# A fused attention and feed-forward kernel: own product copied ahead of the casts, weight casts moved from GpSimd to ScalarE, the product by value from VectorE to GpSimd

## The reference

```python
def reference(q, k, v, tau, moe, moe2):
    qn = q / (norm(q, axis=tokens) + 1e-6); kn = k / (norm(k, axis=tokens) + 1e-6)
    a = softmax(kn.T @ qn / tau)            # 256 x 256
    x = v @ a                               # 6016 x 256
    xn = x / rms(x) * rms_g
    g, val = xn @ w_gate, xn @ w_val        # 256 -> 1536
    y = (g * sigmoid(g) * val) @ w_out      # 1536 -> 256
    h = y @ w_in                            # 256 -> 2048
    return (h - tanh(h)) @ w_out2           # 2048 -> 256
```

## Time and profile before

| | us |
|---|---|
| median of 3 runs (lowest, highest) | 1223.22 (1222.99, 1223.24) |
| profiled execution | 1223.24, its span 1221.4 |
| PE busy | 1179.6 (97%), weight loads 989.7 (81%) |
| VectorE busy | 963.3 (79%) |
| ScalarE busy | 455.1 (37%) |
| GpSimd busy | 262.1 (21%) |
| ScalarE: cast of 512 columns, mean (L861); of 1024 (L743) | 0.611; 1.050 |
| VectorE: low part of 512 columns, mean (L1258) | 0.712 |
| VectorE: seven unit's product by value, mean (L1214); shortest and longest | 1.000; 0.548 and 1.494 |
| GpSimd: gate product (L721), shortest and longest | 1.009 and 1.795 |
| GpSimd: cast of 1024 columns, mean (L714) | 1.225 |
| load of combined weights, 1 MB, from issue to landing, median | 5.3 |

### The profile page before, as it was taken

The page is one execution under the profiler, slowest core; times in us unless marked ns, Lnnn a source line. Parts: engine busy times, 40 slices in busy tenths (PEclk is TensorE's granted clock), DMA queues, the critical chain, the costliest instruction groups (busy, mean ns, idle before and its releaser), DMA issues.

```text
span 1221.4 us, 18368 instructions
## 1 busy us (share of the span) xinstructions
PE 1179.6 (97%) x5858; PEld 989.7 (81%) x5858; DVE 963.3 (79%) x1760; ACT 455.1 (37%) x775; POOL 262.1 (21%) x208
## 2 busy tenths in 40 slices
PE   9999999999999999998999999999999899999999
PEld 8888887877877887887887787788788778888898
DVE  6888797886977877788697697778878869778776
ACT  7866424233322423423332332342342333234232
POOL 4610002042033014113203302401410430330220
PEclk9999999999999999999999999999999999999999
DMA  9524544061043024005104202501510520320300
GB/s 371 188 74 117 146 109 142 1 173 69 1 129 111 0 74 133 33 8 164 69 0 137 103 0 86 155 0 17 187 36 0 163 74 0 121 104 1 91 31 14
DMA packets 132790, 104.83 MB, mean 86 GB/s; under 512 B 90640, under 2 KB 112784, under 8 KB 132752
## 3 DMA queue, kind: packets, MB, share of 16 engines
q1 hardware_dynamic: 132320, 103.83, 27.2%
q10 hardware_dynamic: 432, 0.52, 0.1%
HBM read 91.88 MB, written 12.45 MB: 85 GB/s over the span
## 4 chain that ended last, share of the span: by engine, by line
PE 69%; DVE 15%; issue 7%; ACT 4%; POOL 1%; DMA 1%; DVEq 1%; ACTq 1%; SPq 0%
PE ring L1505 29%; PE out_acc L1563 20%; PE y_acc L1563 6%; PE ring L1556 5%; DVE act L1214 4%; DVE h_lo L1258 2%; PE out_acc L1489 2%; DVE act L1163 2%; PE ring L1521 2%; DVE w_in L1190 2%; PE y_acc L1424 2%; DVE gate_pair L1195 2%; ACT gate_pair L868 1%; PE y_acc L1434 1%; POOL act L721 1%
## 5 line engine op out<-in xcount | busy, mean ns | idle before, releaser
L836 ACT ACTIVATE act<-ring 128x512 f32<-128x512 f32 (+1 forms) x273 | 159.9, 587 | 296.9 <-PE ring L1505 269.3
L1258 DVE TENSOR_TENSOR h_lo<-act,h_hi 128x512 fp32r<-128x512 f32 (+1 forms) x336 | 235.0, 712 | 8.0
L1505 PE MATMUL ring<-y_hi,wl 128*128 128x512 f32 (+1 forms) x712 | 241.2, 385 | 0.0
L1563 PE MATMUL out_acc<-h_hi,wl 128*128 128x512 f32 x704 | 240.0, 389 | 0.3 <-DVE h_lo L1258 0.3
L721 POOL TENSOR_TENSOR act<-gate_pair,act 128x512 f32<-128x512 f32 (+1 forms) x60 | 80.6, 1344 | 732.6 <-ACT act L873 732.6
L714 POOL CAST wl<-landing 128x1024 fp32r<-128x1024 f32 x120 | 143.5, 1225 | 155.6 <-DMA landing<-combined 155.6
L1173 DVE TENSOR_TENSOR act<-ring,act 128x512 f32<-128x512 f32 (+1 forms) x192 | 128.8, 671 | 55.8 <-ACT act L836 54.9
L1563 PEld LDWEIGHTS out_acc<-h_hi,wl 128*128 128x128 f32 x704 | 132.1, 188 | 28.5 <-DVE h_lo L1258 0.7
L1505 PEld LDWEIGHTS ring<-y_hi,wl 128*128 128x128 f32 x712 | 133.4, 188 | 25.6
L1505 PE MATMUL ring<-y_lo,wl 128*128 128x512 f32 (+1 forms) x356 | 137.0, 385 | 0.0
L1563 PE MATMUL out_acc<-h_lo,wl 128*128 128x512 f32 x352 | 136.9, 389 | 0.0
(11 more groups left out here) (230 smaller groups left out, 2014.4 us busy)
## 6 DMA issues: line engine op xcount, KB each, us to landing
landing<-combined SPq DMA_DIRECT2D x60, 1024.0 KB, 5.3
out_dram<-out_rows SPq DMA_DIRECT2D x88, 64.0 KB, 1.8
qk_in<-in_k_dram SPq DMA_DIRECT2D x9, 512.0 KB, 8.8
qk_in<-in_q_dram SPq DMA_DIRECT2D x9, 512.0 KB, 9.8
v_in<-in_v_dram SPq DMA_DIRECT2D x72, 64.0 KB, 2.3
w_in<-in_moe_w_out_dram SPq DMA_DIRECT2D x12, 256.0 KB, 3.0
combined<-wl SPq DMA_DIRECT2D x12, 256.0 KB, 4.2
combined<-w_in SPq DMA_DIRECT2D x12, 256.0 KB, 3.2
```

The lines of the kernel that those rows point to most:

```text
L836: nc.scalar.activation(act[:, u % RING, 0:width], bank(t, name)[:, 0:width], func).then_inc(act_ready, 1)
L1258: nc.vector.tensor_tensor(h_lo[:, u % RING, 0:width], act[:, u % RING, 0:width], f32(h_hi[:, u % RING, 0:width]), ALU.subtract).then_inc(h ...
L1505: ins = nc.tensor.matmul(bank(t, name)[:, 0:width], weights(c, w_part), (hi if part else lo)[:, c, 0:width], start=c == 0 and w_part and part,
L1563: ins = nc.tensor.matmul(acc[:, d, 0:width], weights, (h_hi if part else h_lo)[:, u % RING, 0:width], start=f == 0 and w_part and part, st ...
```

## The change

Three things move.

1. In `seven_unit` ScalarE copies the own product first and casts units p-2 and p-1 after it; until now the cast of the seven unit stood ahead of the next pair's copy. Only in the last pair is the seven unit's cast still behind the sigmoid of the plain unit.
2. `mark_seven` goes from GpSimd to ScalarE, as one instruction over both planes, one seven unit ahead instead of two, between the casts and the sigmoid of `gate_pair`. The first block is cast after tile 1. TensorE waits for one increment instead of two.
3. GpSimd multiplies by gate and then by value (`finish_seven`), and signals `seven_made`. VectorE's second sum (value0) waits for `seven_made` of the pair before, as it overwrites `value_pair`. In the last pair VectorE makes both products itself, ahead of the plain unit's.

```diff
-        PRODUCTS, STEPS, T_STEPS = 7, 8, 4
+        PRODUCTS, STEPS, T_STEPS = 7, 7, 4
+
+        LAST_SEVEN = 2 * SEVENS - 2
...
-            def mark_seven(t, j):
-
-                n = j % len(SEVEN_BLOCKS)
-                pool.wait_ge(seven_loaded[n], t * 32 + (16 * (j // len(SEVEN_BLOCKS) + 1) - 32 * SEVEN_FROM))
-                for low in range(2):
-                    nc.gpsimd.tensor_copy(wl[:, low, SEVEN_BLOCKS[n], :],
-                                          landing[:, low, SEVEN_BLOCKS[n], :]).then_inc(seven_ready, 1)
-
-            def gate_seven(t, p):
+            def finish_seven(t, p):
                 width = width_of(t)
                 buf = act[:, p % RING, 0:width]
                 pool.wait_ge(act_ready, t * U + p + 1)
                 nc.gpsimd.tensor_tensor(buf, gate_pair[:, 0:width], buf, ALU.mult).then_inc(seven_gated, 1)
...
+                pool.wait_ge(seven_gated, sevens(t, p, 1, 1))
+                pool.wait_ge(seven_step, sevens(t, p, STEPS, BY_VALUE0))
+                nc.gpsimd.tensor_tensor(buf, value_pair[:, 0:width], buf, ALU.mult).then_inc(seven_made, 1)
+
+            for t in range(SEVEN_FROM, TILES):
+                for p in range(0, LAST_SEVEN, 2):
+                    finish_seven(t, p)
...
             def cast_any(t, u, width):
 
-                act_e.wait_ge(seven_step, sevens(t, u, STEPS, STEPS)) if u % 2 == 0 else \
+                if u % 2 == 0:
+                    act_e.wait_ge(seven_made, sevens(t, u, 1, 1))
+                else:
                     act_e.wait_ge(bank_free, freed(t, ("value", u)))
...
-            def seven_unit(t, p, width):
+            def mark_seven(t, j):
+
+                n = j % len(SEVEN_BLOCKS)
+                act_e.wait_ge(seven_loaded[n], t * 32 + (16 * (j // len(SEVEN_BLOCKS) + 1) - 32 * SEVEN_FROM))
+                nc.scalar.copy(wl[:, :, SEVEN_BLOCKS[n], :], landing[:, :, SEVEN_BLOCKS[n], :]).then_inc(seven_ready, 1)
+
+            def seven_unit(t, p, width, last):
                 half = width // 2
                 act_e.wait_ge(seven_full, sevens(t, p, PRODUCTS, OWN))
                 if p > 0:
                     act_e.wait_ge(seven_gated, sevens(t, p))
                 nc.scalar.copy(gate_pair[:, 0:half], bank(t, ("own", p))[:, 0:half]).then_inc(own_copied, 1)
-                if p > 0:
-                    cast_any(t, p - 1, width)
+                for u in range(max(p - 2, 0), p):
+                    cast_any(t, u, width)
+                if p < LAST_SEVEN:
+                    mark_seven(t, p // 2 + 1)
+                elif not last:
+                    mark_seven(t + 1, 0)
                 act_e.wait_ge(seven_step, sevens(t, p, STEPS, BY_GATE1))
...
-                        if not is_plain(t):
+                        if not is_plain(t) and f == G - 1:
                             cast_any(t, f - 1, width)
...
             first_tile()
             tile(1, False)
+            mark_seven(SEVEN_FROM, 0)
...
                 dve.wait_ge(seven_full, sevens(t, p, PRODUCTS, SUM3))
+                if p > 0:
+
+                    dve.wait_ge(seven_made, sevens(t, p))
                 nc.vector.tensor_tensor(value0, of("sum3"), u2, ALU.add).then_inc(seven_step, 1)
...
-            def seven_value(t, p, width):
+            def finish_seven(t, p, width):
                 buf = act[:, p % RING, 0:width]
+                dve.wait_ge(act_ready, t * U + p + 1)
+                nc.vector.tensor_tensor(buf, gate_pair[:, 0:width], buf, ALU.mult).then_inc(seven_gated, 1)
                 dve.wait_ge(seven_gated, sevens(t, p, 1, 1))
                 dve.wait_ge(seven_step, sevens(t, p, STEPS, BY_VALUE0))
-                nc.vector.tensor_tensor(buf, value_pair[:, 0:width], buf, ALU.mult).then_inc(seven_step, 1)
+                nc.vector.tensor_tensor(buf, value_pair[:, 0:width], buf, ALU.mult).then_inc(seven_made, 1)
...
                         seven_sums(t, f, width, lambda: low_before(f))
                         beside(f)
+                        if f == LAST_SEVEN:
+                            finish_seven(t, f, width)
                         continue
                     buf = act[:, f % RING, 0:width]
-                    if is_plain(t):
-                        gate_times(t, f, buf, width)
-                    else:
-                        ending = f == G - 1
-                        if ending:
-                            gate_times(t, f, buf, width, lambda: seven_value(t, f - 1, width))
-                            low_unit(t, f - 1, width)
-                        else:
-                            gate_times(t, f, buf, width)
-                            seven_value(t, f - 1, width)
+                    gate_times(t, f, buf, width)
+                    if not is_plain(t) and f == G - 1:
+                        low_unit(t, f - 1, width)
...
-                        pe.wait_ge(seven_ready, sevens(t, f, 2, 2))
+                        pe.wait_ge(seven_ready, sevens(t, f, 1, 1))
```

More of the change, by code:

```diff
@@ L343, in build @@
         seven_gated = sem("seven_gated")
+        seven_made = sem("seven_made")
         seven_step = sem("seven_step")
@@ L721, in gate_seven @@
                 nc.gpsimd.tensor_tensor(buf, gate_pair[:, 0:width], buf, ALU.mult).then_inc(seven_gated, 1)
-            for j in range(len(SEVEN_BLOCKS)):
-                mark_seven(SEVEN_FROM, j)
-            MARKED = len(SEVEN_BLOCKS)
-            for n in range(SEVENS * (TILES - SEVEN_FROM)):
-                gate_seven(SEVEN_FROM + n // SEVENS, 2 * (n % SEVENS))
-                if n > 0:
-                    ahead = n - 1 + MARKED
-                    if ahead < SEVENS * (TILES - SEVEN_FROM):
-                        mark_seven(SEVEN_FROM + ahead // SEVENS, ahead % SEVENS)
+                pool.wait_ge(seven_gated, sevens(t, p, 1, 1))
[4 more added lines that the diff above has]
+                    finish_seven(t, p)
         @block.scalar
@@ L933, in tile @@
                     if is_seven(t, f):
-                        seven_unit(t, f, width)
+                        seven_unit(t, f, width, last)
                     else:
                         nonlinear(t, f, ("gate", f), ACT.Sigmoid, False, width)
-                        if not is_plain(t):
+                        if not is_plain(t) and f == G - 1:
                             cast_any(t, f - 1, width)
@@ L1157, in _, with gate_times @@
             spread_scales(0, TILE)
-            def gate_times(t, f, buf, width, between=lambda: None):
+            def gate_times(t, f, buf, width):
                 gate, value = ("gate", f), ("value", f)
@@ L1163, in gate_times @@
                 nc.vector.tensor_tensor(buf, bank(t, gate)[:, 0:width], buf, ALU.mult).then_inc(bank_free, 1)
-                between()
                 dve.wait_ge(bank_free, freed(t, gate))
```

## The result

The changed kernel takes 1172.53 us (median of 4 runs, 1172.05 to 1172.82), the kernel before beside it 1223.23 (1222.99 to 1223.66, 4 runs). The ratio is 0.9585, 95% interval 0.9568 to 0.9601: 50.7 us faster, where 49.0 were forecast (1174.2, range 1167 to 1184). The profiled execution took 1172.82, its span 1170.7, at the full granted clock throughout.

The account below looks back on a forecast made before the run. TensorE was held by waits on other engines, 6.15 us a tile. 5.42 us in each of eight looped tiles (43.4), 3.6 in tile 10 and 2.0 in the last total 49.0: 1223.22 to 1174.2 us, range 1167 to 1184.

Parts of the forecast that it names:

- Part 1: Own copy ahead of both casts, at +0.55: third to fifth pair 8.0 us long, 3.10 won; second pair 1.13 won.
- the cover before the plain value: VectorE ends gate1 at +4.66, TensorE reaches the plain value at about +5.25: cover of 0.6 us.
- Part 2: Weight casts go from GpSimd to ScalarE as one 1.9 us copy, covered by 0.7 before the sigmoid: zero effect.
- Landing: Fourth block's weights: ScalarE waits 0.2 us, covered; some 2 us later is tolerable; short tile loses perhaps 0.4.
- Part 3: Both products on GpSimd, 1.37 us each; covers 1.7 (next copy), 1.4 (second sum), 0.7 (cast): zero cost.
- the loop that the prediction wrote down: Second sum, sigmoid, two GpSimd products, back: 3.9 + 2x, 6.6 us at x = 1.37; binds past 2.05.
- Part 4: Last pair, VectorE keeps both products: low parts come before TensorE wants them, cover 0.3, so 1.19 us goes entirely.
- A: More won in the second pair or first pair's short waits, up to 6.15 a tile: 55.5 us, 1167.7; chance 0.12.
- B: Another engine uses up a cover, 0.5 lost in four pairs of ten tiles: 20 us back, 1194; chance 0.15.
- C: GpSimd held off VectorE's port on both products, each past 2.5 us: 24 us more, 1247; chance 0.04.
- D: TensorE gains nothing though waits go, since VectorE turns up elsewhere: 1223; chance 0.02.
- E: Product by value on the path, GpSimd's 0.69 more paid in each of 50 pairs: 34 us back, 1208; chance 0.03.

Follow-up runs that it names:

- Part 1 alone: The kernel before with only ScalarE's own copy put ahead of both casts; weight casts stay on GpSimd, the product by value on VectorE: 1193.25 us, ratio 0.9748.
- the two placements: The changed kernel with weight casts back on GpSimd, made either behind VectorE's low parts (1176.26 us) or beside them in four pairs (1204.22 us).
- the kernel with the late landing: The changed kernel with VectorE's second transposition of output rows moved behind the second pair's low parts: 1200.27 us, ratio 0.9808.

## Why the prediction was right

**Part 1: right to a few hundredths.** Third to fifth pair 8.00 each (about 8.0 forecast; 3.19 us won for 3.10, though 27.19 less three times the prediction's own 8.0 is 3.19 already), copy at +0.62 (0.55), wait for the third sum gone. The second pair was forecast at 8.50 - 1.13 = 7.37 and lasts 7.31, sums at +1.60 instead of +1.67. Part 1 alone is worth 31.0 us on the kernel before, and 31.6 when taken from the kernel after. One term was too large: the cover before the plain value is 0.25, not 0.6, since gate1 ends at +4.81 instead of +4.66, and the loader wants it at +5.06, 0.2 ahead of the product itself (which is at +5.28, 5.25 forecast). Nothing ran into it in this kernel.

**Part 2: the cost right, the worth missed.** The cast of 2048 takes 1.908 us, 1.9 was taken from the square; it is covered, by 0.90 in the third pair. The Trainium skill (ScalarE: Activation LUTs, What ACT_TABLE_LOAD costs) has 186 ns + 0.833 ns per column for an ACTIVATE with immediate scale and bias, which gives an estimate of 1.89 us here; the trace agrees for this cast within 1%. But the prediction booked the removal from GpSimd at nothing. It had a row of such a meeting, two low parts at 2.42 beside GpSimd's gate product, and used it only to ask where new overlaps would come, not what becomes of the casts if part 1 comes alone. In the kernel before, the cast of the fourth block missed the low parts of the third pair, ending at 358.62 before they began:

```profile
359.03 1.28 DVE L1258 TENSOR_TENSOR h_lo<-act,h_hi 128x512 fp32r<-128x512 f32 x2
```

The two low parts ahead of gate0 took 1.28 there in every such pair of the looped tiles. Part 1 moves them earlier against the landing, and they meet the casts: 2.13 us in tile 3 with part 1 alone (casts from 352.74 to 355.23, low parts from 353.64). Only 0.25 us stands ahead of the plain value, and casts left on GpSimd overrun that. So part 2 is worth 16.9 us once parts 1, 3 and 4 are in, shown by undoing it and, for the cause, by the two placements. That its missing worth did no harm to the forecast is in part luck: the sum was built against TensorE's floor, and the change happened to contain the part that is needed to reach it.

**Landing.** For a full tile the 0.2 us wait forecast did not cost anything; with the transposition later, a wait of 4.35 did, as "up to some 2 us later" had warned. In the short tile the margin was taken too lightly: 0.4 was the term, and the third pair lasts 7.38 where its products need 6.53. The lines of the kernel after:

```profile
1108.33 1.91 ACT L860 CAST wl<-landing 128x2048 fp32r<-128x2048 f32 x1 [2.70 <-DMA landing<-combined]
1110.14 0.52 ACT L876 ACTIVATE act<-gate_pair 128x384 f32<-128x384 f32 x1
...
1111.82 0.32 ACT L867 COPY gate_pair<-ring 128x192 f32<-128x192 f32 x1 [0.79 <-POOL act L716]
```

The late cast delays the sigmoid, this GpSimd's gate product, this the next copy. The last tile gave 1.1 us instead of 2.0.

**Part 3: right.** The covers of the two products hold: 0.87 us of extra delay cost 0.3, 2.73 cost 56.9, by the loop that the prediction wrote down. VectorE's product gone is worth 5.5 us (0.6 in each tile), which stood inside the 1.13 of the second pair.

**Part 4: right in size, its own share not shown.** 12.09 for 12.1, and the 1.19 went entirely. From the last own copy of tile 3 to the first of tile 4 it takes 58.90 us before and with part 1 alone, 58.25 after, and 58.24 with the product by value back on VectorE in the first five pairs. With the weight casts on GpSimd it takes 59.22, or 58.64 behind the low parts. So part 2 is needed for it as well, and the rest falls to part 4 by exclusion, as no run undoes that alone.

**The sum.** Forecast per looped tile 5.42, measured 5.54 in tile 2 and 5.62 on the mean in the others: 44.9 for 43.4. Tile 10: 3.97 for 3.6. The last: 1.14 for 2.0. Ahead of tile 2: 0.7, nothing of which the change touches but a cast; the other kernels here show their first copy between 240.1 and 241.3, and one at 243.0, so I count it as scatter.

**The rivals.** A's further gain, the rest of the second pair, is real but needs another edit (4.6 us, by moving transposition and load). B's mechanism is real and was kept out by part 2: the kernel with casts beside the low parts is B's loss in four pairs, some 8.6 us for a pair and 1.7 more in the last, 31.7 us over after where B had 20. C needs over 2.5 us for a GpSimd product, and was reached with 2.7 us of spare work; the gate product's mean after the change is 1.394, its longest 1.80. D and E are refuted, by the span and by the kernel with the product on VectorE.

## What to carry to other kernels

When an engine queue holds a step that waits for a far result ahead of a step that everybody waits for, put the latter first: that order alone was worth 31 us of 1224. When an edit moves a step earlier, ask again what other engines do beside it; casts on GpSimd that had missed VectorE's low parts met them then and cost 15 to 17 us, and less than 4 when they were moved by some two microseconds. Measure a cover to the moment when the weight loader would go on; here it was 0.25 us and not 0.6. A transposition that gates a store also gates every load behind that store in the queue.

## What the runs showed of the hardware

- GpSimd's cast of 1024 float32 columns and VectorE's low part, which reads two SBUF operands, slow each other: two low parts take 1.28 us alone and 2.12 to 2.38 beside the casts, two casts 2.03 alone and 2.88 beside the low parts. VectorE's sums, which read PSUM, stayed at 0.41 to 0.42 beside them. VectorE's products of two SBUF operands took 1.00 to 1.41 beside the casts for 0.69 alone.
- A chain of GpSimd casts of 256 columns does less to VectorE: 1.48 to 1.66 for the two low parts. It costs GpSimd 3.92 / 7 = 0.56 us each there, and 0.87 / 2 = 0.44 or 2.73 / 6 = 0.46 elsewhere.
- GpSimd's gate product of 512 columns took 1.53 us in the second pair, where a low part ran beside its start, and 1.30 in the third; its product by value took 1.29 on the mean. In the kernel before it took 1.29 while two low parts beside it took 2.42.
- TensorE's granted clock fell only in the kernel with the late landing, after waits of the loader: in tile 7 it stood idle for 1.61, 0.98 and 0.40 us in a row, and the wide products then came 0.43 us apart instead of 0.23 (granted clock 0.81 from 745 to 754).
